# Twelve groups of unread TensorE products, each with another order of reading, at the end of a convolution and feed-forward kernel

## The reference

```python
# attn: softmax over 7 taps for each of 8 heads, then a causal weighted sum over 7 rows
w = exp(weight_gen - max); w = w / (sum(w) + 1e-9)
out = einsum('bshk,bskhg->bshg', w, x_unfolded)      # (2, 4096, 192) -> 8192 tokens x 192
# first feed-forward
h = maximum(x @ w_in, 0);  x = (h * h) @ w_out        # 192 -> 2048 -> 192
# second feed-forward
h = x @ w_in2;  g = h * cos(h);  out = g @ w_out2     # 192 -> 2048 -> 192
```

## Time and profile before

| | |
|---|---|
| median of 2 runs | 1177.7 us (1177.59 to 1177.81) |
| the profiled execution, device time | 1177.56 us |
| its span, first to last instruction | 1175.7 us |
| TensorE busy | 1172.7 us, 9953 products |
| VectorE, ScalarE, GpSimd busy | 960.4, 806.1, 366.3 us |
| TensorE's granted clock | 1.000 of full speed |

### The profile page before, as it was taken

How to read it: one execution, slowest core, us unless ns; L and a number is a source line. 1 busy time by engine, 2 the same in 40 slices (tenths; PEclk the granted TensorE clock), 3 DMA queues, 4 the chain that set the end, 5 groups by cost and what they waited for, 6 DMA issues and landing times.

```text
span 1175.7 us, 25787 instructions
## 1 busy us (share of the span) xinstructions
PE 1172.7 (100%) x9953; PEld 1132.5 (96%) x9954; DVE 960.4 (82%) x1504; ACT 806.1 (69%) x1467; POOL 366.3 (31%) x265
## 2 busy tenths in 40 slices
PE   9999999999999999999999999999999999999999
PEld 7989999999999999999999999999999999999988
DVE  7968899878878787887878878787787878878787
ACT  4977666667667666666766666676666767666676
POOL 4993634070420706125070430705215070000000
DMA  8511111110111101111011111101111000100001
GB/s 214 135 51 30 35 28 35 17 37 15 23 35 28 35 11 19 35 28 35 15 19 34 25 35 28 35 9 21 35 28 35 13 17 3 26 2 15 1 1 28
DMA packets 113174, 37.33 MB, mean 32 GB/s; under 512 B 101662, under 2 KB 110878, under 8 KB 113052
## 3 DMA queue, kind: packets, MB, share of 16 engines
q1 hardware_dynamic: 111100, 34.87, 14.2%
q10 hardware_dynamic: 1952, 0.80, 0.3%
HBM read 23.84 MB, written 6.29 MB: 26 GB/s over the span
## 4 chain that ended last, share of the span: by engine, by line
PE 100%; issue 0%; DVE 0%
PE y L608 51%; PE h L608 46%; PE y L713 1%; PE h L630 1%; PE h L1121 0%; PE h L637 0%; PE y L674 0%; PE h L640 0%; PE h L644 0%; PE h L1123 0%; PE y L675 0%; PE y L676 0%; PE y L725 0%; DVE g_hi L1543 0%; PE y L659 0%
## 5 line engine op out<-in xcount | busy, mean ns | idle before, releaser
L608 PE MATMUL y<-g_hi,wo 64*128 64x512 f32 x3048 | 698.2, 393 | 0.2
L608 PE MATMUL y<-g_lo,wo 64*128 64x512 f32 x2032 | 521.1, 391 | 0.0
L608 PEld LDWEIGHTS y<-g_hi,wo 64*128 64x128 f32 x3048 | 420.5, 184 | 14.5 <-PE y L608 1.1
L529 POOL TENSOR_TENSOR tap<-xc,gen 128x768 f32<-128x768 f32 x98 | 150.9, 1546 | 575.3 <-DVE xd_lo L1522 555.2
L608 PEld LDWEIGHTS y<-g_lo,wo 64*128 64x128 f32 x2032 | 305.3, 184 | 2.0
L1179 ACT ACTIVATE turns<-turns 128x512 f32<-128x512 f32 x238 | 150.2, 631 | 182.4 <-DVE turns L1473 182.4
L608 PE MATMUL h<-xa_hi,wa_hi 64*128 64x512 f32 x1018 | 270.6, 397 | 0.1
L608 PE MATMUL h<-xa_hi,wa_lo 64*128 64x512 f32 x1018 | 266.0, 391 | 0.0
L608 PE MATMUL h<-xa_lo,wa_hi 64*128 64x512 f32 x1018 | 265.5, 391 | 0.0
L1493 DVE TENSOR_TENSOR h<-h,turns 128x512 f32<-128x512 f32 x238 | 165.6, 696 | 114.6 <-ACT turns L1179 114.2
L1467 DVE SCALAR_TENSOR_TENSOR h<-h,relu 128x512 f32<-128x512 f32 x249 | 173.4, 696 | 57.2 <-ACT relu L1154 55.0
(11 more groups left out here) (127 smaller groups left out, 1092.7 us busy)
## 6 DMA issues: line engine op xcount, KB each, us to landing
xc<-in_x_dram SPq DMA_DIRECT2D x60, 240.0 KB
out_dram<-arena SPq DMA_DIRECT2D x62, 64.0 KB, 1.9
xt_a<-x_blocks SPq DMA_DIRECT2D x224, 16.0 KB, 1.8
arena<-in_moe_w_out_dram SPq DMA_DIRECT2D x16, 192.0 KB, 3.7
arena<-in_moe_w_in_dram SPq DMA_DIRECT2D x16, 128.0 KB, 2.5
out_dram<-arena SPq DMA_DIRECT2D x62, 32.0 KB, 1.7
xt_d<-x_blocks SPq DMA_DIRECT2D x112, 16.0 KB, 1.8
arena<-in_moe_w_in_dram SPq DMA_DIRECT2D x16, 64.0 KB, 2.9
```

The costliest lines, as they stand in the source:

```text
L529: pool.tensor_tensor(tap[:, k % 2, :].rearrange("p (r g) -> p r g", g=GROUP), rows[k], wk, ALU.mult).then_inc(pool_step, 1)
L608: return pe.matmul(o, w[rows, :], x[rows, :], start=start, stop=stop)
```

## The change

The sixteen unread products at the end become forty-eight: twelve orders, four products of each, all of float32r with a 128 x 128 stationary and 512 moving elements. The moving operand is no longer `g2_hi` but the weights `wo[1]`, so is the stationary operand (slots 8 to 11 of it). They write the four banks of `h` in turn. Nothing else is changed.

```diff
-            spare = g2_hi[:, 0, :]
-            line = spare[:, 0:4].unsqueeze(1).to_broadcast([P, TOK // 4, 4])
-            pairs = spare.rearrange("p (b n two) -> p n b two", b=2, two=2)
-            lines = spare.rearrange("p (b n four) -> p n b four", b=2, four=4)
-            for j, moving in enumerate((line, pairs, lines)):
-                for _ in range(4):
-                    pe.matmul(h[:, j, :], wo[1][:, j, 0:P], moving, start=True, stop=True)
-            for _ in range(4):
-                pe.matmul(h[:, 3, :], wo[1][:, 3, 0:DD].bitcast(mybir.dt.bfloat16),
-                          spare[:, 0:TOK // 2].bitcast(mybir.dt.bfloat16), start=True, stop=True)
+            flat = wo[1][:, :, :].rearrange("p f d -> p (f d)")
+            even = flat[:, 0:TOK]
+            far = flat.rearrange("p (b n) -> p b n", b=2)[:, :, 0:TOK // 2]
+            orders = [
+                even,
+                flat[:, 4:TOK + 4],
+                flat[:, 1:TOK + 1],
+                even.rearrange("p (n k four) -> p k n four", k=2, four=4),
+                even.rearrange("p (n k four) -> p k n four", k=8, four=4),
+                even.rearrange("p (n k four) -> p k n four", k=32, four=4),
+                far.rearrange("p b (n four) -> p n b four", four=4),
+                even.rearrange("p (b n run) -> p n b run", b=2, run=8),
+                even.rearrange("p (b n run) -> p n b run", b=2, run=16),
+                even.rearrange("p (b n run) -> p n b run", b=2, run=32),
+                even[:, 0:TOK // 2].rearrange("p (n four) -> p n four", four=4).unsqueeze(2).to_broadcast(
+                    [P, TOK // 8, 2, 4]),
+                even.rearrange("p (b n four) -> p n b four", b=4, four=4),
+            ]
+            for j, moving in enumerate(orders):
+                for k in range(4):
+                    pe.matmul(h[:, j % 4, :], wo[1][:, 8 + k, 0:P], moving, start=True, stop=True)
```

## The result

The changed kernel takes **1184.61 us** (median of 2 runs, 1184.49 to 1184.73) against 1177.7; the ratio is 1.0059, with a 95% interval of 1.0043 to 1.0076. The forecast was 1184.5. The profiled execution took 1184.49 with a span of 1182.7 at a granted clock of 1.000.

The account below looks back on a forecast made before the run. TensorE was taken to bound the kernel, the stores ending it almost in a tie; 48 products at 11.56 us from 1170.58 end the span at 1182.52, +6.8 us on 1177.7, so 1184.5 us, range 1183.6 to 1187.0.

Parts of the forecast that it names:

- What ends the program: At the program's end: almost a tie, the output stores coming about 0.45 us after TensorE.
- The 0.45 us: Behind TensorE's old tail: the first 0.45 us of a longer tail costs nothing, the rest lengthens the program one to one.
- The first start: First unread product after line 688: stays at 1170.58 us, moved by nothing.
- The sum of the 48: TensorE's new tail: four products of each of twelve orders, 11.56 us in all, the last starting at 1181.89.
- order 4: New tail, four elements at a time with steps of 32 bytes: 0.250 us a product, bounds 0.218 and 0.330.
- order 11: New tail, each four elements read twice: 0.225 us a product, the middle of 0.218 and 0.233.
- orders 6 and 12: New tail, four elements at a time with steps of 512 bytes: 0.250 us a product, bounds 0.218 and 0.330.
- The third sign: New tail: the forecast is wrong if the order shifted by 4 bytes (0.235 us) is not priced as side by side (0.233).
- The meeting of the engines: After the last product: 0.02 us for the drain's end and 0.2 us until the last event.
- free orders: Rival, new tail: order does not matter, all 48 cost 0.233 us, 11.18 us, time 1184.1; chance 0.25.
- The second rival: New tail: step distance or 16-byte border matters, such orders priced like the pairs, 0.330 us; dear orders given chance 0.20.
- Contention: New tail beside the output stores' DMA traffic: no slowing of the reads, given nothing either way.

Follow-up runs that it names:

- experiment 1: Kernel before without any of its unread products at the end: 1177.65 us, ratio 1.000 (0.999 to 1.001).
- experiment 8: Sixteen groups of six unread products, four elements at a time, steps 256 to 1088 bytes, read by starts: with 16 places 283 ns at 256, 234 at 272.
- experiments 2 and 3: 48 unread products all side by side, replacing the kernel before's sixteen: 1183.97 us; the changed kernel with its twelve orders reversed: 1184.60 us.

## Why the prediction was right

- **What ends the program**: held, but the room was mis-sized. That the stores end the old program was read from the waits, and experiment 1 shows it: without the products the time is the same. The 0.45 us, though, was counted to the end of SyncE's wait at 1175.3; SyncE's own drain follows only at 1175.5. From the last product's end to the end of the span it was 0.92 us before and is 0.25 now, so 0.67 us of the longer tail cost nothing. The sum did not use the 0.45: it added 0.22 to the last product's end and so took about 0.7 for free.
- **The first start**: 1170.58 forecast, 1170.68 measured. The other kernels that differ only in the tail had 1170.43 to 1170.88, so the body varies by that much between executions.
- **The sum of the 48**: the last product starts 11.34 us after the first, where 11.56 - 0.25 = 11.31 were forecast. Four orders were off and cancelled: order 4 by -19 ns, order 11 by -9, orders 6 and 12 by +17 each; 5 and 7 to 10 were off by -4 to +4. The cancelling was luck, but not what the forecast hung on: the dear two alone would have added 0.14 us, the cheap two alone taken 0.11 away. What was wrong is the mechanism. I had priced all steps alike, and said that the forecast is wrong if a step's distance changes the price; it does, from 231 at 32 bytes to 267 at 512. By these runs a step counts by its place modulo 256 (experiment 8), which no row of the old trace could show: its one step was 1 KiB, a multiple of 256, with two places. The third sign, order 3 priced unlike order 1, did not show beyond 3 ns (236 and 233).
- **The meeting of the engines**: forecast 0.22 behind the last product's end, measured 0.25 (1182.44 to 1182.69).
- **Rivals**: free orders (1184.1) fell by the prices of 240 to 267, and 48 side by side did take less, 1183.97. The second rival had the better mechanism, that the distance of a step matters and that round distances come back to the same place, but not the price: 330 was forecast, and the dearest cost 285 in any run with four at a time. (By its own prices one or two dear orders give 1184.8 to 1185.2, not 1184.9 to 1185.3.) Slower by over 2% would have needed 770, and single elements 48 bytes apart at 637 are the dearest of all that was tried.
- **Contention**: the conclusion held, its ground did not. The cheapest group had ended at 1171.45, before the stores' traffic, and the bfloat16 products began at 1174.01, in the stretch with the DMA engines at 0.33 and not at 0.90. It is experiments 2 and 3 that show it: beside the traffic the prices by order were the same as behind it.
- **What a measurement can tell**: 2% was taken for the limit. The interval of the ratio is 1.0043 to 1.0076, so a rise of 0.6% is clear of no change.
- Single elements with a step of 8 bytes, two on each 16-byte line, cost 462 ns, no less than the 461 with one on each. The rule from the Trainium skill (Advanced Engine Details and Errata, SBUF Cachelines) that two hits on a line absorb the access latency does not hold here.

## What to carry to other kernels

Read TensorE's moving operand in pieces of at least 16 bytes, and if it must change places, avoid steps that are multiples of 256 bytes (up to 285 against 232 ns for 512 float32r elements). With 4 and 16 places a step with 16 to 64 bytes more is free (227 to 235 ns). With two places, look at the jump back too: 16 bytes more changed nothing (251), 64 bytes more gave 240. In a kernel that TensorE bounds, look where the moving and the stationary operands begin modulo 256 bytes: moving the first by 224 bytes gave 1.4% here. To price an addition at a program's end, look first at what else is still running there, and count only what outlasts it.

## What was not expected of the hardware

- Side by side, float32r products came to 227 ns only where the operands' beginnings agree modulo 256 bytes, and stayed at 229 to 235 in the other groups. Each four read twice, each two twice and each one twice all take 216, the distance of the bfloat16 products. A lighter weight load changes nothing.
- Single elements cost about double from a step of 8 bytes on (462), not more at 32 (432), but 637 at 48 bytes; why is open.
- Left open: why two places 1 KiB apart with eight, sixteen and thirty-two elements at a time cost 243, 240 and 237 while four places with eight at a time cost 231, and why 128 bytes cost 245 to 253. Neither has two reads of 16 bytes in a row that agree modulo 256. Open too is why steps of 64 bytes cost 225 to 227.
